# The last 64 rows of a dense layer's low-part product: from a whole array to half of it, two column blocks at a time

## The reference

```
h = x @ w_in
g = np.maximum(0.01 * h, h)
return g @ w_out
```

## Time and profile before

| | before |
|---|---|
| median of 3 runs | 822.89 us (820.84 to 823.64) |
| profiled execution | 821.72 us |
| its span, first to last instruction | 820.0 us |
| TensorE matmul busy | 748.0 us (91%) |
| TensorE weight load busy | 554.9 us (68%) |
| VectorE busy | 518.3 us (63%) |
| ScalarE busy | 415.9 us (51%) |
| mean granted TensorE clock | 0.97 |

### The profile page before, as it was taken

One profiled execution on the slowest core, in us unless ns is written; L12 is line 12 of the kernel. 1 busy time (PEld: TensorE's weight loads), 2 busy tenths in 40 slices (PEclk: granted clock), 3 DMA queues, 4 the chain that ended last, 5 costly groups with the idle time before them and its releaser, 6 DMA issues.

```text
span 820.0 us, 17971 instructions
## 1 busy us (share of the span) xinstructions
PE 748.0 (91%) x6435; PEld 554.9 (68%) x6436; DVE 518.3 (63%) x1346; ACT 415.9 (51%) x811; POOL 192.4 (23%) x286
## 2 busy tenths in 40 slices
PE   4899999993697989799999899999999999999994
PEld 3688889882486878687888756556565555565552
DVE  7868898997876545565567665555465455554441
ACT  4578777778652266554656223343443433434332
POOL 4468787782311001010100000020010100100101
PEclk9999999997798989999999999999999999999997
DMA  6889979732415974478330000000000000000000
GB/s 198 225 233 298 335 239 318 226 128 80 127 59 215 354 253 147 162 282 338 109 139 0 2 1 1 1 33 1 1 33 1 33 0 0 32 0 0 33 2 32
DMA packets 35879, 95.77 MB, mean 117 GB/s; under 512 B 7102, under 2 KB 19582, under 8 KB 33246
## 3 DMA queue, kind: packets, MB, share of 16 engines
q1 hardware_dynamic: 28434, 63.71, 24.6%
q10 hardware_dynamic: 4732, 22.10, 7.5%
q0 software_dynamic: 2640, 9.01, 3.3%
HBM read 70.92 MB, written 23.89 MB: 116 GB/s over the span
## 4 chain that ended last, share of the span: by engine, by line
PE 79%; DVE 5%; ACT 5%; DMA 4%; issue 4%; SPq 1%; POOL 1%; ACTq 0%; DVEq 0%; POOLq 0%
PE bank L1669 33%; PE bank L1806 19%; PE bank L1703 10%; PE bank L1532 4%; PE bank L1556 4%; DMA stage<-wA 2%; ACT xw L777 1%; PE bank L1578 1%; PE bank L1542 1%; PE bank L1548 1%; PE bank L1659 1%; DMA slot<-qkT 1%; DMA d_x<-og 1%; PE bank L1522 1%; PE bank L1524 1%
## 5 line engine op out<-in xcount | busy, mean ns | idle before, releaser
L1669 PE MATMUL bank<-stage,slot 128*128 128x512 f16 x768 | 181.1, 379 | 0.0
L1806 PE MATMUL bank<-slot,dec 128*128 128x320 f16 x768 | 159.1, 299 | 0.0
L1669 PE MATMUL bank<-qbd,slot 128*128 128x128 f16 x1984 | 122.5, 225 | 13.7 <-issue 9.3
L1669 PEld LDWEIGHTS bank<-qbd,slot 128*128 128x128 f16 x1984 | 118.4, 101 | 17.2 <-issue 16.8
L1669 PEld LDWEIGHTS bank<-stage,slot 128*128 128x128 f16 x768 | 75.1, 98 | 74.3 <-DVE stage L1464 0.3
L1468 DVE TENSOR_TENSOR qk<-stage,dec 128x512 f16<-128x512 f32 x96 | 66.4, 692 | 85.1 <-ACT dec L964 85.1
L1806 PE MATMUL bank<-slot,qk 128*128 128x320 f16 x384 | 114.8, 299 | 0.0
L964 ACT CAST dec<-stage 128x512 f16<-128x512 f32 x96 | 59.4, 619 | 101.1 <-PE bank L1806 74.5
L693 POOL DMA_INDIRECT out<-stage,tok_i x24 | 23.6, 983 | 369.5 <-ACT stage L975 365.6
L1464 DVE TENSOR_TENSOR stage<-bank,stage 128x512 f32<-128x512 f32 x96 | 66.2, 690 | 67.0 <-ACT stage L958 66.0
L958 ACT ACTIVATE stage<-bank 128x512 f32<-128x512 f32 x96 | 57.3, 597 | 97.2 <-PE bank L1669 96.2
(11 more groups left out here) (268 smaller groups left out, 1187.6 us busy)
## 6 DMA issues: line engine op xcount, KB each, us to landing
slot<-d_w SPq DMA_DIRECT2D x12, 1280.0 KB, 6.5
d_w<-slot ACTq DMA_DIRECT2D x4, 2560.0 KB, 11.2
stage<-wB SPq DMA_DIRECT2D x6, 1280.0 KB, 9.0
stage<-wA SPq DMA_DIRECT2D x6, 1024.0 KB
d_w<-slot SPq DMA_DIRECT2D x4, 1280.0 KB, 8.3
stage<-wB ACTq DMA_DIRECT2D x4, 1280.0 KB, 13.2
qk<-qkT SPq DMA_DIRECT2D x12, 360.0 KB, 5.9
slot<-qkT SPq DMA_DIRECT2D x12, 360.0 KB, 7.8
```

The costliest lines, as they stand in the source:

```text
L1669: ins = t_.matmul(pf, a[:, col:col + P], x(k), start=(q == 0), stop=(q == len(ops) - 1))
L1806: ins = t_.matmul(bank[4 + q][:, 0:DM], x[f % 2][:, q * P:(q + 1) * P], slotB[2 + f // NF][:, c0:c0 + DM], start=(f == 0 and z == 0), stop ...
```

## The change

For the two dense weight units the block k = 2 is kept in another way. For the even hidden units (half 0 of the columns) nothing changes: high part in rows 0 to 63, low part in rows 64 to 127. For the odd ones (half 1) it is the other way round: low part in rows 0 to 63, high part in rows 64 to 127. `low` does this with two instructions of 64x512 in the place of one of 64x1024.

The 16 blocks are taken in another order, by `block_at`: an even f is a block of even hidden units, f + 1 the block of odd ones at the same place. The last of the 8 matmuls of a block is taken out of `f_first` into `f_first_end`. It now contracts over 64 rows only, the high weight part times the low token part: rows 0 to 63 for an even f, rows 64 to 127 for an odd one. The product of the low weight part with the low token part for k = 2 is no longer computed. TensorE's order is now first product f, first product f + 1 (7 matmuls each), the two halves, and then the second products f - 2 and f - 1, with a turn behind the one at which it stood before. The orders of ScalarE, VectorE, POOL and the DMA queues are as before.

```diff
--- before.py
+++ after.py
@@ -1122,6 +1122,12 @@
                 sc = wsc[:, u:u + 1, k // 3]
                 if k == 2:
                     sc = wsc[KR:P, u:u + 1, 0]
+                if k == 2 and y >= NE:
+                    w, x = by_chunk(slotA[t][:, 2 * FE:3 * FE]), by_unit(part(y % 2, k))
+                    v.scalar_tensor_tensor(w[0:KR, 1, :], x[0:KR, 1, :], wsc[0:KR, u:u + 1, 0], w[0:KR, 1, :],
+                                           ALU.mult, ALU.subtract)
+                    o_ = h_ = w[KR:P, 0, :]
+                    x = x[KR:P, 0, :]
                 v.scalar_tensor_tensor(o_, x, sc, h_, ALU.mult, ALU.subtract).then_inc(lo_done, 1)
 
             def weigh(u, g, i):
@@ -1784,14 +1790,24 @@
                                        ident[:, :])
                 ins.then_inc(f_tr, 1)
 
+            def block_at(f):
+                return f // 2 % (NF // 2) + f % 2 * NF // 2
+
             def f_first(gr, f, i):
                 w = gr * 2 * NF + f
                 if not (isinstance(w, int) and w < 2):
                     pe.wait_ge(f_g, w - 1)
                 if f == 0:
                     pe.wait_ge(f_yl, (gr + 1) * GT)
-                first(slotA[2 + f // NF], lambda k: yh[i][:, k, :], lambda k: yl[i][:, k, :],
-                      bank[f % 2][:, :], f % NF, 512).then_inc(f_h, 1)
+                a, at, lo = slotA[2 + f // NF], block_at(f) * P, 3 * FE
+                for q, (col, x, k) in enumerate([(at, yh, 0), (lo + at, yh, 0), (at, yl, 0), (FE + at, yh, 1),
+                                                 (lo + FE + at, yh, 1), (FE + at, yl, 1), (2 * FE + at, yh, 2)]):
+                    t_.matmul(bank[f % 2][:, :], a[:, col:col + P], x[i][:, k, :], start=(q == 0), stop=False)
+
+            def f_first_end(f, i):
+                at, r = 2 * FE + block_at(f) * P, f % 2 * KR
+                t_.matmul(bank[f % 2][:, :], slotA[2 + f // NF][r:r + KR, at:at + P], yl[i][r:r + KR, 2, :],
+                          start=False, stop=True).then_inc(f_h, 1)
 
             def f_second(gr, f):
                 w = gr * 2 * NF + f
@@ -1802,22 +1818,26 @@
                     if f == 0 and not (isinstance(gr, int) and gr == 0):
                         pe.wait_ge(f_ob, (gr - 1) * GT + q + 1)
                     for z, (x, hl_) in enumerate(((fhi, 0), (fhi, 1), (flo, 0))):
-                        c0 = (2 * (f % NF) + hl_) * DM
+                        c0 = (2 * block_at(f) + hl_) * DM
                         ins = t_.matmul(bank[4 + q][:, 0:DM], x[f % 2][:, q * P:(q + 1) * P],
                                         slotB[2 + f // NF][:, c0:c0 + DM], start=(f == 0 and z == 0),
                                         stop=(f == 2 * NF - 1 and z == 2))
                     ins.then_inc(f_o, 1)
 
             def group(gr, i, prep):
-                for f in range(2 * NF):
+                for f in range(0, 2 * NF, 2):
                     f_first(gr, f, i)
-                    if f < 2 and not (isinstance(gr, int) and gr == 0):
-                        f_second(gr - 1, 2 * NF - 2 + f)
-                    if f >= 2:
-                        f_second(gr, f - 2)
-                    if prep and f - TURN in PREP_AT:
-                        q = PREP_AT.index(f - TURN)
-                        y_turn((gr + 1) * GT + q, q)
+                    f_first(gr, f + 1, i)
+                    f_first_end(f, i)
+                    f_first_end(f + 1, i)
+                    for n in range(f, f + 2):
+                        if n < 2 and not (isinstance(gr, int) and gr == 0):
+                            f_second(gr - 1, 2 * NF - 2 + n)
+                        if n >= 2:
+                            f_second(gr, n - 2)
+                        if prep and n - TURN in PREP_AT:
+                            q = PREP_AT.index(n - TURN)
+                            y_turn((gr + 1) * GT + q, q)
 
 
             pe.wait_ge(m_xl, NPAIR)
```

## The result

The changed kernel takes 831.04 us (median of 20 runs, 823.79 to 834.14) against 823.66 us for the one before (20 runs, 820.84 to 827.13). The ratio is 1.0085, with a 95% interval of 1.0067 to 1.0103, so the change costs 7 us. The forecast was 831, slower.

A forecast was written before the change was run, and what follows sets the result against it. TensorE was taken to bound the kernel, busy without a gap in the dense stage. -10.4 + 12.0 + 4.2 + 2.1 + 0.4 = +8.3 us gave a forecast median of 831 us, own range 828 to 837.5, full range 819 to 839.

The forecast's parts named there:

- Saved slots, -10.4: Dense stage on TensorE: halves stream side by side, saving one 0.216 us slot in each of 48 pairs, -10.4 us.
- Price of the half height, +12.0 (low end 8.6): TensorE entering and leaving half height: 0.25 us per pair, 48 pairs, +12.0 us; low end 0.18 per pair, +8.6.
- the delay of the second half: Second half's weights load after the first's, in each pair: bounds 0.01 and 0.10 us, taken as 0.05.
- the ten fp32 transposes: 32-row transposes between 120- and 128-row matmuls in the trace before; the prediction read 0.10 us in and 0.10 out there.
- Ten gaps at the scales, +4.2: Even blocks f = 4 and 10 of five groups: scale work on VectorE delays the second maximum, 0.42 us each, +4.2.
- Start +2.1, end +0.4: Dense stage ends: TensorE gaps of 1.64 and 0.50 us at the start, second product 15 late at the end.
- Nothing at the other places: Scale work after f = 1, 7, turns at f = 6, 12 and group starts: claimed hidden, no TensorE gap.
- The two `low` instructions of 64x512: VectorE, expert stage: +0.1 us for each of two weight units, claimed hidden under TensorE's work, taken as 0.
- The signs of being wrong: Prediction wrong if the pair period is below 6.58 us, or if TensorE's forecast waits for VectorE's maximum are missing.
- a change of height is free (819): Rival, chance 0.20: changing height costs nothing with these shapes, so -10.4 + 6.7 of stalls = -3.7, 819.2 us.
- the halves don't overlap (839): Rival, chance 0.12: halves run one after the other, a pair saves nothing and pays 0.20, +16.3, 839 us.
- the order costs nothing (824.5): Rival, chance 0.10: the new block order brings no stalls of 6.7 us, so -10.4 + 12.0 = +1.6, 824.5 us.

The follow-up runs named there:

- the experiment: Changed kernel with the next group's scales worked out at blocks 1, 5, 7, 11 in place of 1, 4, 7, 10: 825.6 us, ratio 1.0021.
- the second experiment: Kernel before, old order and layout, with each dense block's last matmul over rows 0 to 63 only, one at a time: 843.03 us, ratio 1.0243.
- the third: Changed kernel with both halves of a pair in rows 0 to 63, weights laid out as before: 838.43 us, ratio 1.0198.
- the first: Changed kernel's block order with all matmuls at full height, weights and `low` as in the kernel before: 830.46 us, ratio 1.0092.
- first version: Changed kernel taken four blocks at a time, turns at blocks 6, 7, 10, 13: 842.89 us with halves, 846.81 us with all matmuls whole.

## Why the prediction was right, point by point

- **Saved slots, -10.4.** Right: 0.21 per pair by the halves in the same rows against the halves in different rows, 10.1 us; by the distance of starts in the changed kernel 0.213 per pair, 10.2 us. The side-by-side streaming had no row in the trace of before and was assumed; it is shown now.
- **Price of the half height, +12.0 (low end 8.6).** The mechanism was right, the size too high: 0.210 per change in and out, 10.1 us. The mis-sized term is the delay of the second half, taken as 0.05; both start within 5 ns. The 0.10 in and 0.10 out, read off the ten fp32 transposes, were right for fp16 matmuls of 512 columns: 0.10 in, 0.10 out and 0.01 for the load that was not done ahead.
- **Ten gaps at the scales, +4.2.** 4.9 by the timeline and 5.0 by the experiment: a little too small. The subtraction starts 0.72 after the cast there, not 0.66. The trace of before already has 0.72 to 0.75 at all 20 places where `y_top` comes between the maximum and the subtraction, and 0.65 to 0.68 at all others; the prediction took its offset from one of the others.
- **Start +2.1, end +0.4.** 2.12 and 0.34 in the timeline. But the gap of 1.64 already holds the first pair's 0.10 of going back, which the sum also has in its price: counted once it is 2.0. Taking both ends away gave 2.0 us, the 2.35 less a wait of 0.39 that came back at the second pair.
- **Nothing at the other places.** Right: no wait of TensorE at f = 1, 6, 7 or 12. The two `low` instructions of 64x512 take 1.54 us from the first's start to VectorE's next instruction, where the one of 64x1024 took 1.32: 0.2 for each weight unit, and not the 0.1 forecast. The start of the dense stage doesn't show this among its own spread.
- **Sum.** +8.3 forecast, +7.24 in the stage. The price was 1.9 too high and the gaps 0.7 too small; the exit counted twice (-0.1) and the saved slots (+0.2) make up the rest. That the forecast median of 831 fits to 0.04 us is luck: the change was forecast 1 us too large, and the median of before was 823.66 rather than the 822.9 of the three runs shown. The signs of being wrong did not come: a pair takes 6.71 us, not below 6.58, and the waits are there.
- **The rivals.** That a change of height is free (819) fell with the second experiment, that the halves don't overlap (839) with the third, that the order costs nothing (824.5) with the first.

## What to carry to other kernels

Where an engine is busy without a gap, price a saved slot against what it takes to reach it: here 0.21 us to go into half height and back, for 0.21 us saved. Such a price is paid per change, so gather the small matmuls behind one change before judging the idea; two blocks at a time gave nothing, four gave 5.1 us, 0.6%. The four blocks also took four banks and two more buffers of each kind, and in their first version the order cost 25 us: look for the stalls of the new order before giving up the idea.

Two first products in a row make both banks due soon after each other, with the engines behind them one after the other in between. Write out, from the moment when both are ready, when each engine of the chain starts and what stands ahead of it in its own order; the slow place is the one where odd work stands between the two.

## What the runs showed of the hardware

- Two matmuls over rows 0 to 63 and 64 to 127 into two banks start within 5 ns of each other (two records of 386 ns within 0.39 us) and stream together; in the same rows the second starts 0.22 us later. The Trainium skill, "TensorE: Matmul & The Clock Gate", section "Part 3: Packing small matmuls", gives about 4 ns from the start of one tile to the next; the trace agrees, with its 5 ns at most.
- Going from full height to 64 rows costs 0.10 us after the last column has streamed, and going back 0.10 to 0.11, whether one half, two or four stand between; the weight load does not run ahead across the change. The Trainium skill, "TensorEngine Tiling (Array Packing)", section Key Properties, says that a change of the tiling mode drains TensorE, without a time. The trace agrees in that both changes cost, 0.21 us together.
- 96 rows cost nothing, as the 120 of the attention stage: 96 such matmuls made the stage 0.4 us longer, in one run. Whether any other height below 128 but 64 and the transposes' 32 has the price was not tried.
- The granted clock fell to 1.2 GHz in the stage only where TensorE had waited long: in the first versions by fours, behind waits of 2.5 to 2.7 us, and there not behind every one (two of five and three of five). In the changed kernel, whose longest wait is 1.65 us, it was 1.00 throughout the stage.
